# The mask of the local attention scores added by TensorE for all head pairs, not for the first four alone

## The reference

```python
mask = np.abs(pos[:, None] - pos[None, :]) < factor        # factor = 4
scores = scale * np.matmul(q, k.transpose(0, 1, 3, 2))
scores = np.where(mask, scores, -1000000000.0)
scores = scores - np.max(scores, axis=-1, keepdims=True)
attn = np.exp(scores)
attn = attn / (np.sum(attn, axis=-1, keepdims=True) + 1e-09)
out_local = np.matmul(attn, v)
...
h = x @ w_in
g = h * np.clip(h + 3.0, 0.0, 6.0) / 6.0
x = g @ w_out
...
h = np.maximum(np.maximum(x @ w1, x @ w2), x @ w3)
return h @ w_out
```

## Time and profile before

| | |
|---|---|
| median of 3 runs | 812.91 us (812.9 to 813.33) |
| profiled execution | 814.86 us, span 813.1 us |
| mean granted TensorE clock | 0.993 |
| TensorE matmuls busy | 797.0 us, 98% of the span |
| VectorE busy | 310.7 us |
| ScalarE busy | 277.1 us |
| GpSimd busy | 163.1 us |

### The profile page before, as it was taken

One profiled execution on the slowest core, in us unless ns is written; L12 is line 12 of the kernel. 1 busy time (PEld: TensorE's weight loads), 2 busy tenths in 40 slices (PEclk: granted clock), 3 DMA queues, 4 the chain that ended last, 5 costly groups with the idle time before them and its releaser, 6 DMA issues.

```text
span 813.1 us, 12702 instructions
## 1 busy us (share of the span) xinstructions
PE 797.0 (98%) x5346; PEld 661.6 (81%) x5346; DVE 310.7 (38%) x602; ACT 277.1 (34%) x619; POOL 163.1 (20%) x196
## 2 busy tenths in 40 slices
PE   8789999999999999999999999999999999999998
PEld 6577777878787887888888899888888888888897
DVE  6555565355445654553323234233022113112211
ACT  5655555444344433433323256222112112111111
POOL 8655756321022112110000038100000000000000
PEclk9899999999999999999999999999999999999999
DMA  9972422122211321110200066100110020010010
GB/s 174 206 219 73 135 62 61 34 85 55 61 32 30 113 61 32 30 31 11 94 1 0 1 186 205 52 0 1 40 64 1 27 79 0 14 65 0 14 40 27
DMA packets 93477, 49.06 MB, mean 60 GB/s; under 512 B 61164, under 2 KB 84204, under 8 KB 93420
## 3 DMA queue, kind: packets, MB, share of 16 engines
q1 hardware_dynamic: 90740, 47.36, 21.2%
q10 hardware_dynamic: 2680, 0.89, 0.6%
HBM read 38.79 MB, written 9.44 MB: 59 GB/s over the span
## 4 chain that ended last, share of the span: by engine, by line
PE 92%; SPq 3%; POOL 2%; ACT 1%; DVE 1%; DMA 1%; issue 0%
PE bank L691 29%; PE bank L693 28%; PE bank L692 28%; PE bank L826 2%; PE bank L748 1%; PE bank L803 1%; PE bank L765 1%; PE bank L792 1%; PE bank L778 1%; POOL w L641 1%; SPq L415 1%; DMA w_raw<-in_moe_w_out_dram 1%; POOL dp_a L633 1%; PE bank L710 1%; SPq L465 1%; PE bank L720 0%
## 5 line engine op out<-in xcount | busy, mean ns | idle before, releaser
L691 PE MATMUL bank<-xs,w 128*128 128x512 f32 (+1 forms) x680 | 253.1, 372 | 0.0
L693 PE MATMUL bank<-xs,w 128*128 128x512 f32 (+1 forms) x680 | 250.4, 368 | 0.0
L692 PE MATMUL bank<-xs,w 128*128 128x512 f32 (+1 forms) x680 | 250.3, 368 | 0.0
L691 PEld LDWEIGHTS bank<-xs,w 128*128 128x128 f32 x680 | 128.2, 189 | 22.1 <-issue 1.0
L693 PEld LDWEIGHTS bank<-xs,w 128*128 128x128 f32 x680 | 128.2, 189 | 21.6
L692 PEld LDWEIGHTS bank<-xs,w 128*128 128x128 f32 x680 | 128.3, 189 | 20.6
L691 PE MATMUL bank<-gs,w 128*128 128x512 f32 (+1 forms) x320 | 121.7, 380 | 0.8 <-DVE gs L1389 0.8
L1382 DVE SCALAR_TENSOR_TENSOR rg<-rg,bank 128x512 f32<-128x512 f32 (+1 forms) x80 | 50.7, 633 | 177.5 <-ACT rg L1098 177.5
L692 PE MATMUL bank<-gs,w 128*128 128x512 f32 (+1 forms) x320 | 118.0, 369 | 0.0
L693 PE MATMUL bank<-gs,w 128*128 128x512 f32 (+1 forms) x320 | 118.0, 369 | 0.0
L1098 ACT ACTIVATE rg<-bank,half 128x512 f32<-128x512 f32 (+1 forms) x80 | 51.6, 646 | 176.6 <-PE bank L693 176.6
(11 more groups left out here) (211 smaller groups left out, 826.4 us busy)
## 6 DMA issues: line engine op xcount, KB each, us to landing
w_raw<-in_moe_w_out_dram SPq DMA_DIRECT2D x22, 256.0 KB, 4.4
w_raw<-in_moe_w_dram SPq DMA_DIRECT2D x18, 256.0 KB, 3.2
out_dram<-o_sb SPq DMA_DIRECT2D x18, 256.0 KB, 2.0
w_raw<-in_moe_w_in_dram SPq DMA_DIRECT2D x16, 256.0 KB, 3.7
x_scratch<-y SPq DMA_DIRECT2D x4, 1024.0 KB, 4.8
xr<-x_scratch SPq DMA_DIRECT2D x4, 1024.0 KB, 6.4
q_nat_a<-in_q_dram SPq DMA_DIRECT2D x26, 144.0 KB, 2.9
v_a<-in_v_dram SPq DMA_DIRECT2D x24, 144.0 KB
```

What stands on the lines that cost most here:

```text
L691: mm(dst, w[0], m[0], start=start, stop=False, skip_group_check=True)
L692: mm(dst, w[0], m[1], start=False, stop=False, skip_group_check=True)
L693: return mm(dst, w[1], m[0], start=False, stop=stop, skip_group_check=True)
```

## The change

TensorE writes the mask for all pairs, and VectorE's max_local and sub_local are now the old max_masked and sub_masked for all. mask_local, the tensor mask, its laying by GpSimd and the semaphores s_mask and s_madd go. scores_down waits for s_lsub (the subtraction) for all pairs, where for pairs 4 to 15 it waited for s_madd (the masking). maskb and identb move to memory that is kept.

```diff
-    mask = work("mask", [P, 2, TPH, KW])
+
+    maskb = work("maskb", [P, 2, TPH, KW], BF16)
+    identb = work("identb", [P, P], BF16)
...
-            lay_mask(mask, lambda h, x, t: mask[x * KW:(x + 1) * KW, h, t, :], s_mask)
...
                 pe.wait_ge(s_cqk, 4 * n + 4)
-                if n < PAIRS:
-
+
+                if n == 0:
                     pe.wait_ge(s_mb, 1)
                     pe.wait_ge(s_idb, 1)
-                    for x in range(2):
-                        for h, dst in enumerate((t.ba, t.bb)):
-                            rows = slice(h * KW, (h + 1) * KW)
-                            mm(dst[x * KW:(x + 1) * KW, 0:TPH * KW], identb[rows, rows],
-                               maskb[rows, x].rearrange("p t w -> p (t w)"), start=True, stop=False,
-                               skip_group_check=True)
+                for x in range(2):
+                    for h, dst in enumerate((t.ba, t.bb)):
+                        rows = slice(h * KW, (h + 1) * KW)
+                        mm(dst[x * KW:(x + 1) * KW, 0:TPH * KW], identb[rows, rows],
+                           maskb[rows, x].rearrange("p t w -> p (t w)"), start=True, stop=False,
+                           skip_group_check=True)
...
-                                      t.kT[rows, a:a + KW], start=n >= PAIRS, stop=True, skip_group_check=True)
+                                      t.kT[rows, a:a + KW], start=False, stop=True, skip_group_check=True)
...
-                if n < PAIRS:
-                    pe.wait_ge(s_lsub, n + 1)
-                else:
-                    pe.wait_ge(s_madd, 2 * (n - PAIRS) + 2)
+                pe.wait_ge(s_lsub, n + 1)
...
-                    vec.tensor_tensor(t.lp[:, h], src[:, 0:TPH * KW].rearrange("p (t w) -> p t w", w=KW),
-                                      mask[:, h], ALU.add).then_inc(s_madd, 1)
...
-                vec.tensor_reduce(t.lnm[:], lp, AX, ALU.max, negate=True).then_inc(s_lmax, 1)
...
-                vec.tensor_tensor(lp, lp, t.lnm[:].unsqueeze(2).to_broadcast([P, 2 * TPH, KW]),
-                                  ALU.add).then_inc(s_lsub, 1)
...
                     if i == STAGES[1]:
-                        mask_local(n)
                         max_local(n)
                         sub_local(n)
```

More of the change, by code:

```diff
@@ L184, in work @@
     def work(name, shape, dt=F32, line=32):
-        size = 4
+        size = 2 if dt == BF16 else 4
         for n in shape[1:]:
@@ L268, in attention_moe_kernel @@
         work_c = working("_c", 3, 4)
-        maskb = work("maskb", [P, 2, TPH, KW], BF16)
-        identb = work("identb", [P, P], BF16)
         mask_raw = work_c.lp
@@ L320, in attention_moe_kernel @@
         s_ident = sem("s_ident")
-        s_mask = sem("s_mask")
         s_mraw = sem("s_mraw")
@@ L335, in attention_moe_kernel @@
         s_sl = sem("s_sl")
-        s_madd = sem("s_madd")
         s_lmax = sem("s_lmax")
@@ L1256, in pool_qk @@
                                   AX, ALU.add).then_inc(s_pool, 1)
[L1258 to L1262, removed]
-                    vec.tensor_tensor(t.lp[:, h], src[:, 0:TPH * KW].rearrange("p (t w) -> p t w", w=KW),
-                                      mask[:, h], ALU.add).then_inc(s_madd, 1)
-            def max_local(n):
-                t = tiles(n)
-                dve.wait_ge(s_madd, 2 * (n - PAIRS) + 2)
-                lp = t.lp[:].rearrange("p h t w -> p (h t) w")
-                vec.tensor_reduce(t.lnm[:], lp, AX, ALU.max, negate=True).then_inc(s_lmax, 1)
[L1273 to L1277, removed]
-                vec.tensor_tensor(lp, lp, t.lnm[:].unsqueeze(2).to_broadcast([P, 2 * TPH, KW]),
-                                  ALU.add).then_inc(s_lsub, 1)
-            def max_masked(n):
+            def max_local(n):
                 t = tiles(n)
@@ L1290, in max_masked, with sub_local @@
                 mine.then_inc(s_lmax, 1)
-            def sub_masked(n):
+            def sub_local(n):
                 t = tiles(n)
@@ L1418, in _ @@
             pool_qk(0)
-            max_masked(0)
-            sub_masked(0)
+            max_local(0)
+            sub_local(0)
             pool_qk(1)
@@ L1423, in _ @@
             inverse_local(0)
-            max_masked(1)
+            max_local(1)
             inverse_down(0)
-            sub_masked(1)
-            max_masked(2)
+            sub_local(1)
+            max_local(2)
             inverse_local(1)
@@ L1430, in _ @@
             pool_qk(2)
-            sub_masked(2)
+            sub_local(2)
             inverse_down(1)
@@ L1437, in _ @@
             pool_qk(3)
-            max_masked(3)
+            max_local(3)
             inverse_down(2)
-            sub_masked(3)
+            sub_local(3)
             max_down(3)
```

## The result

The changed kernel takes 815.92 us (median of 16 executions, 814.0 to 819.45), the kernel before 813.53 (16 executions). The ratio is 1.0031, 95% interval 1.0019 to 1.0042: 2.5 us, 0.3% slower, by more than the 0.2% that can be told from no change. The forecast was 814.1, range 812.9 to 815.7. The profiled execution took 817.85 us, its span is 816.1. Single executions of either kernel spread over 4 to 5 us, about 0.5%, much wider than the three times shown before. Executions more than 1.5% over the fastest of their kernel are left out of the medians (one of 3841 us in e3_wait_only, one of 1115 us of the kernel before).

A forecast was written before the change was run, and what follows sets the result against it. The prediction took TensorE's own work to bound the kernel. Eleven pairs by 0.105 us and pair 4 at 0 gave +1.15 us on the 812.91 us median: 814.1 us, range 812.9 to 815.7.

The forecast's parts named there:

- What bounds the kernel: Whole kernel: TensorE, busy in 98% of the span, sets the time; VectorE's other maskings lie hidden.
- 0.105 us a pair: TensorE, pairs 4 to 15: net price of four mask matmuls before the scores, bounds 0.05 to 0.16 us.
- Pairs 5 and 7 hide the longer wait: Coarse scores of these tight pairs: twelve large matmuls cover VectorE's 1.81 us, 0.4 us left, cost 0.
- Pair 4 about 0: Pair 4: coarse scores 1.02 us later, absorbed by a 1.01 us wait at turn_down; at most 1.0 us.
- The clock rival: Behind pair 4's scores: a gap of about 2.1 us halves the clock, adding 1.7 us, 815.8 us; chance 0.13.
- Nothing in the SP queue moves: SP queue: the change moves nothing there; listed under what costs nothing.
- The end of the start: First large matmul of hidden(1): stays in place; the forecast is wrong if it moves.
- The price theory: From the follow-ups, not the prediction: mask matmuls and their effect on neighbours make up all of the 2.4 us.
- the clock theory: From the follow-ups: matmuls cost 0.14 us a pair, 1.5 us; pair 4's longer gap sometimes drops the clock for 3.4 us.

The follow-up runs named there:

- e3_wait_only: The kernel before, with the coarse scores waiting for VectorE's subtraction for all pairs and no added mask matmuls; 816.84 us, ratio 1.0042.
- e7: The changed kernel with each mask of pairs 4 to 15 written twice, eight mask matmuls a pair; 817.13 us, ratio 1.0044.
- e8: The changed kernel with the mask matmuls of pairs 4 to 15 cut from 320 to 64 columns; 814.53 us, ratio 1.0010.
- e9: The changed kernel with the four mask matmuls in another order, both of one head first; 816.91 us, ratio 1.0047.
- c1: The kernel before, with a new order around pair 4 on TensorE, GpSimd and ScalarE; 812.19 us, ratio 0.9985.
- e4: The changed kernel, but pair 4 alone masked by VectorE the old way, its coarse scores waiting for that masking; 814.66 us, ratio 1.0011.
- e1: The changed kernel with 17 idle matmuls of 256 columns between pair 4's local and coarse scores; 815.68 us, ratio 1.0020.
- e2: The changed kernel with VectorE also masking pairs 4 to 15 as before, and the coarse scores waiting for that masking; 816.39 us, ratio 1.0026.
- e5: The changed kernel with the coarse scores of pair 4 behind add_out(1) instead of in front of it; 815.20 us, ratio 1.0021.
- c2: The changed kernel with a new order around pair 4 on TensorE, GpSimd and ScalarE; 812.80 us, ratio 0.9992.

## Why the prediction was wrong

The direction was right and the size was not: +1.15 us, called no measurable change, against 2.4 to 2.5 us over the series before, and 815.92 us is 0.2 us above the range. The second series of the same kernel has 815.44 us, 1.9 over the kernel before and inside the range, so how far the number misses is partly scatter. The sum behind it is short all the same, of a part of one term and of two terms that it put at nothing. Point by point:

- **What bounds the kernel**: right. VectorE's busy time went down by 8.5 us (9.6 forecast) and GpSimd's by 6, and none of it showed in the time.
- **0.105 us a pair**: the step that was mis-sized. Its own two terms held, 0.16 us ahead of the scores and 0.84 us in all. But it ended at the next large matmul, and the twelve behind it lose another 0.041 us. The term is 0.140, eleven times 1.54 us where 1.16 was forecast. The start could not show this, since no large matmuls stand behind the scores there.
- **Pairs 5 and 7 hide the longer wait**: right, no wait there. In e3, where VectorE's chain is the old one, both wait about 0.5 us.
- **Pair 4 about 0**: right, even pessimistic, when the clock stays: 19.71 us against 19.96.
- **The clock rival, 0.13, 1.7 us**: the mechanism was right, its price (1.6 measured) too, and its chance was far too low. Six traces have a gap of 2.0 us or more at pair 4 (the changed kernel twice, e3, e7, e8, e9), and the clock fell behind it in four. Eight have no such gap, and it fell there in none. The times of single executions bear it out. An execution with a mean granted clock of 0.997 or more has about 3.4 us at half clock and no more, and every trace has at least that much in its start, at 28 to 37 us. Of the six series with the gap 6 of 67 executions are of this kind, of all others whose clock is on record 69 of 179. The mean of the granted clock gives a smaller share. The 56 executions of the five series with the 2.0 us gap have 0.9947, the 179 without a gap 0.9954. The difference of 0.0007 is about a third of one fall (3.4 us at half clock in 813 is 0.0021). So the term is 0.55 us by this and 1.1 by the traces, on average over executions. For the changed kernel alone (0.9949 in 28 executions, against 0.9951 in 107 of the kernel before) the mean is too coarse to show it. The forecast put the term at nothing, since it treated the fall as a case apart, which happens or not, where it is a chance in every execution.
- **Nothing in the SP queue moves**: right for the issue, wrong in what lands. From pair 6 to pair 7 the kernel before takes 24.79 us in both traces. The changed one takes 25.49 and 25.17, of which 0.14 is the matmuls, and 0.56 and 0.24 the K of pair 7: the second of its two transfers lands as TensorE asks for it, or after. It is issued 1.11 us behind the start of values_down(6) in all fourteen traces. In five (the two of the kernel before, c1, e3, e4) it lands 2.8 to 3.2 us later and costs nothing. In the nine others, all with the mask on TensorE, it lands 3.7 to 4.35 us later and costs 0.05 to 0.7 us. These nine have a 16 KB packet of the queue q8, "instruction", 0.7 to 1.6 us behind the issue, while K is on its way. In the five it comes 4.6 to 5.0 us behind, when K has landed. The DMA view of the changed kernel, 127 to 132.5 us, and of the kernel before, 126 to 131 us (packets, MB, share; below them issues, KB each, us to landing):

```profile
q8 instruction: 1, 0.02, 1.4%
...
k_nat_a<-in_k_dram SPq DMA_DIRECT2D x2, 144.0 KB, 3.4
```

```profile
q1 hardware_dynamic: 2216, 0.55, 48.8%
q14 instruction: 1, 0.01, 0.4%
...
k_nat_a<-in_k_dram SPq DMA_DIRECT2D x2, 144.0 KB, 2.9
```

- **The end of the start**: it was to stay, and the traces can't tell. turn_q(4) begins at 54.91 and 54.51 us in the changed kernel, between the 55.50 and 52.72 of the kernel before.

Without the clock, the sum of what the traces show is 1.54 − 0.25 + 0.4 (late K) = 1.7 us. The executions with a mean clock of 0.997 or more agree. Their one stretch at half clock is, by all fourteen traces, in the start, so none is left for pair 4: the changed kernel has 5 of them, median 814.16 us, the kernel before 36, median 812.41, a difference of 1.75. With 0.55 to 1.1 us for the clock it is 2.25 to 2.8 us, against 2.4 to 2.5 measured in the first series and 1.9 in the second. The price theory falls: the matmuls cost 1.54 us in every trace of this form, and never more. What the medians of e1 (0.2 us under the changed kernel) and of e2 (0.5 over it) say against the clock theory lies within their scatter, but they don't support it either.

Open stays why four mask matmuls of 320 columns slow the large ones behind by 0.041 us when eight of 320 and four of 64 don't. Columns, count, order and VectorE's reads are excluded. Open too is whether the packet is what holds up K of pair 7: the timing parts all fourteen traces the same way, but no kernel was made for this. That the mask moves the packet is likely: there are 42 such packets for TensorE's 10692 matmuls and weight loads, about one to 255, and the mask adds eight to each pair. And whether the change moves the start by some tenths of a us stays open.

## What to carry to other kernels

The price of instructions put into a full engine is measured from one landmark before them to one well behind them, not to the next instruction: here 0.041 of 0.140 us lay in the neighbours. A wait that grows on the engine that bounds the kernel has two prices, the wait itself and a chance that the clock falls behind it; where no trace shows a fall (1.1 us here) the second is nothing, where some do (2.0 us here) its average belongs in the sum. And a wait is removed only when the next one on its chain is too: e5 gained nothing, c1, which moved three engines together, gained 1.2 us.

## What the runs showed of the hardware

- The granted clock fell behind idle stretches of 2.0 us in three of five traces (of the changed kernel in one of two), behind one of 2.8 us in the only trace that has it, and behind none of 1.1 us between large matmuls (in the start, with small ones around, a stretch with a wait of 1.0 us had a fall behind it in six of fourteen traces, as in the earlier trace rows). It stayed at half for 3.4 us each time at pair 4.
- Four matmuls of 64 by 64 by 320 in bf16 in four quarters of the array take 0.16 us together, eight take 0.30.
- The slowdown of 0.041 us in twelve large matmuls is the same to a nanosecond in each of the pairs 5 to 15 of seven kernels (the changed one, e1, e2, e4, e5, e9, c2).
- A K transfer of 144 KB took 2.8 to 3.2 us to land in the five traces where no 16 KB packet of the "instruction" queue started meanwhile, and 3.7 to 4.35 us in the nine where one did.
